# A linear-attention and two-network kernel: the last state update of the first planned body is moved to the border of two bodies

## What is computed

```python
k_n = k / (norm(k) + 1e-06)
for t in range(S):                      # S = 768
    y[:, :, t] = q[:, :, t] @ state
    v_old = k_n[:, :, t] @ state
    state = state + beta[t] * outer(k_n[:, :, t], v[:, :, t] - v_old)
h = x @ w_in                            # x: 3072 tokens x 384, w_in: 384 x 2048
g = where(h >= 1, h, where(h <= -1, 0, (h + 1) ** 2 / 4))
x2 = g @ w_out                          # 2048 x 384
xn = x2 / sqrt(mean(x2 * x2) + 1e-6) * rms_g
out = (silu(xn @ w_gate) * (xn @ w_val)) @ w_out2   # 384 x 1536 twice, 1536 x 384
```

## Time and profile before

| | us |
|---|---|
| median of 3 runs | 1040.0 |
| lowest and highest | 1039.98, 1040.58 |
| the profiled execution | 1040.48 |
| its span on the core | 1038.7 |
| PE busy in it | 1023.1 |
| DVE busy | 571.2 |
| ACT busy | 446.0 |

### The profile page before, as it was taken

The page is one execution under the profiler, slowest core; times in us unless marked ns, Lnnn a source line. Parts: engine busy times, 40 slices in busy tenths (PEclk is TensorE's granted clock), DMA queues, the critical chain, the costliest instruction groups (busy, mean ns, idle before and its releaser), DMA issues.

```text
span 1038.7 us, 25028 instructions
## 1 busy us (share of the span) xinstructions
PE 1023.1 (98%) x11080; PEld 845.6 (81%) x11080; DVE 571.2 (55%) x1098; ACT 446.0 (43%) x784; POOL 9.9 (1%) x19
## 2 busy tenths in 40 slices
PE   9999989999999999999999999999999999999998
PEld 4598888777777777777888888888888888888886
DVE  6878859778678777943466444234234333333322
ACT  7754645645544544553576442232232232232121
POOL 1000000000000000000000000000000000000000
PEclk9999999999999999999999999999999999999999
DMA  9204024013212402301512220200100100100101
GB/s 327 94 18 169 3 64 160 16 33 108 99 22 76 140 3 52 104 3 33 183 31 63 90 92 1 61 1 20 42 1 31 31 1 1 31 1 1 31 0 31
DMA packets 31211, 58.85 MB, mean 57 GB/s; under 512 B 2752, under 2 KB 21056, under 8 KB 29696
## 3 DMA queue, kind: packets, MB, share of 16 engines
q1 hardware_dynamic: 30656, 56.47, 17.5%
q10 hardware_dynamic: 448, 0.79, 0.3%
HBM read 43.88 MB, written 13.37 MB: 55 GB/s over the span
## 4 chain that ended last, share of the span: by engine, by line
PE 94%; ACT 2%; DVE 2%; issue 1%; DMA 1%; ACTq 0%
PE bank L805 22%; PE hps L1469 20%; PE acc L1487 19%; PE acc L833 11%; PE hps L805 7%; PE hps L833 4%; PE acc L1515 2%; PE bank L1347 1%; PE bank L1376 1%; PE bank L1395 1%; PE bank L1403 1%; PE bank L1421 1%; PE bank L1438 1%; PE bank L1335 1%; PE bank L1365 1%
## 5 line engine op out<-in xcount | busy, mean ns | idle before, releaser
L713 ACT ACTIVATE g<-bank 128x512 f32<-128x512 f32 x72 | 43.1, 599 | 242.1 <-PE bank L805 129.0
L1469 PE MATMUL hps<-xh,w1h 128*128 128x512 f32 (+1 forms) x336 | 127.7, 380 | 2.2 <-DVE g L1279 2.1
L1487 PE MATMUL acc<-g1h,w2h 128*128 128x512 f32 (+1 forms) x336 | 127.1, 378 | 0.4 <-issue 0.4
L1469 PE MATMUL hps<-xl,w1h 128*128 128x512 f32 (+1 forms) x336 | 122.0, 363 | 0.0
L1487 PE MATMUL acc<-g1l,w2h 128*128 128x512 f32 (+1 forms) x336 | 121.9, 363 | 0.0
L1487 PE MATMUL acc<-g1h,w2l 128*128 128x512 f32 (+1 forms) x336 | 121.8, 363 | 0.0
L1469 PE MATMUL hps<-xh,w1l 128*128 128x512 f32 (+1 forms) x336 | 121.8, 362 | 0.0
L1083 ACT ACTIVATE g1h<-g 128x512 fp32r<-128x512 f32 (+1 forms) x112 | 63.9, 571 | 128.2 <-DVE g L1279 113.0
L1074 ACT ACTIVATE g<-hps,half_c 128x512 f32<-128x512 f32 (+1 forms) x112 | 69.5, 621 | 68.7 <-PE hps L1469 67.3
L1287 DVE TENSOR_TENSOR g1l<-g,g1h 128x512 fp32r<-128x512 f32 (+1 forms) x112 | 68.4, 611 | 48.9 <-ACT g1h L1083 48.6
L1279 DVE SCALAR_TENSOR_TENSOR g<-hps,g 128x512 f32<-128x512 f32 (+1 forms) x112 | 68.2, 609 | 40.8 <-ACT g L1077 40.3
(11 more groups left out here) (238 smaller groups left out, 2026.7 us busy)
## 6 DMA issues: line engine op xcount, KB each, us to landing
kqT<-kq SPq DMA_DIRECT2D x11, 1024.0 KB, 7.1
v_in<-v SPq DMA_DIRECT2D x6, 768.0 KB, 5.3
k_in<-k SPq DMA_DIRECT2D x6, 768.0 KB, 5.3
x2d<-x2s SPq DMA_DIRECT2D x18, 256.0 KB, 5.5
x2t<-x2d SPq DMA_DIRECT2D x6, 768.0 KB, 5.4
y<-y_t SPq DMA_DIRECT2D x44, 96.0 KB, 2.2
x2d<-prob SPq DMA_DIRECT2D x20, 192.0 KB, 2.9
v_in<-x2d SPq DMA_DIRECT2D x10, 384.0 KB, 3.3
```

Source lines behind the costliest of these rows:

```text
L713: act.activation(silu[:, f % 2, :], gps[f % 2][:, :], ACT.Silu).then_inc(e_silu, 1)
L1469: last = pe.matmul(hps[f % 2][:, 0:WIDTH[n]], wt[:, kk, P * f:P * f + P], xx[:, kk, COLS[n]], start=(kk == 0 and e == 0), stop=(kk == KD - ...
L1487: last = pe.matmul(acc[j][:, 0:WIDTH[n]], wt[:, f, P * j:P * j + P], gg[:, f % 2, 0:WIDTH[n]], start=(f == 0 and e == 0), stop=(f == NF1 - ...
```

## The change

In body 1 the last unit of the chain, `KU 1 1`, is taken out of the even steps and given the due time 0.995, which is later than the last of the 192 groups. The remaining 17 units run from `lead` to 0.91 instead of 18 from `lead` to 0.89. In body 2 the two `GQ` units get the due times 0 and 0.09 instead of 0.04 and 0.09. `Z 1 1` and what follows it in body 1 stand 2.93 groups apart instead of 2.55. No instruction is added or removed. In body 2 the units from `Z 2 0` on stand 2.62 groups apart instead of 2.71; bodies 3 to 5 have the list they had.

```diff
--- before.py
+++ after.py
@@ -169,12 +169,15 @@
         at += w / (DENSE if k > 1 else 1.3 * LEAD if at * total < 36 else LEAD if turned is None else 2.5 * LEAD)
         if e == ("xd", k, 1):
             turned = at
-    lead, last = (turned, LAST - 0.02) if k == 1 else (at, LAST)
+    lead, last = (turned, LAST) if k == 1 else (at, LAST)
     us = solve(k) + serial(k)
+    if k == 1:
+        us.remove(("KU", k, HALVES - 1))
+        ev.append((0.995, ("KU", k, HALVES - 1)))
     if k == 1:
         ev += [((done + 68 + 10 * hf) / total, ("GQ", k, hf)) for hf in range(HALVES)]
     else:
-        ev += [(0.04 + 0.05 * hf, ("GQ", k, hf)) for hf in range(HALVES)]
+        ev += [((0.09 * hf if k == 2 else 0.04 + 0.05 * hf), ("GQ", k, hf)) for hf in range(HALVES)]
     begin = None
     for n, u in enumerate(us):
         ev.append((lead + (last - lead) * n / len(us), u))
```

## The result

| us | before | after |
|---|---|---|
| median | 1040.0 (5 runs, 1039.68 to 1041.07) | **1046.58** (5 runs, 1044.49 to 1047.23) |
| the profiled execution | 1040.48 | 1044.49 |
| its span | 1038.7 | 1042.7 |

The ratio is 1.0057, with a 95% interval of 1.0046 to 1.0068: slower, as forecast, but by 6.6 us where 2.8 were forecast, and outside the range of 1040.8 to 1045.0. The profiled execution is the fastest of the five. One execution lost 4.0 us against the profile of before, the median of five lost 6.6; both have to be explained.

A forecast was written before the change was run, and what follows sets the result against it. The prediction took PE as the bound, busy 1023.1 of 1038.7 us. Its terms, 4.1 - 2.1 + 0.35 + 0.7 = +3.05, rounded down to +2.8 on the median 1040.0, gave 1042.8 us, range 1040.8 to 1045.0.

The forecast's parts named there:

- The gap: Between `KU 1 1` and `GQ 2 0`: PE idles until the state addition, 4.1 us, bounds 2.45 and 4.9.
- The load: Output of `PU 1 1` coming back into `v_in`: store to load takes 3.3 us, arriving 8.0 after `PU 1 1`, holding `XE`.
- The clock: Rival, behind the idle time before `GQ 2 0`: the clock falls to half, losing 1.8 us more, 1044.6 us; chance 0.20.
- what it took back: Body 1: the new order costs +0.35 us by a longer wait before `U 1 1` and +0.7 by shifted code borders.
- The wider steps: Body 1: three groups of cover remove waits of 0.34, 0.38, 0.71, a 0.29 border and 0.4 of small things, -2.1 us.
- pairs side by side and to modelled ends: Small things in the gain: one unit edge of 0.19 less, idle times some 0.07 short each; 0.4 us, bounds 0 and 0.6.
- U 1 1: Before `U 1 1`: DVE has `sys` first, so the wait is 0.8 instead of 0.37; +0.35 us, bounds 0 and 0.8.
- the border after `KS 1 1` opens: Code border after `KS 1 1`, hidden so far, begins to cost; part of the upper bound of +1.5 us on code.
- The code borders: `GK 2 0`, `KS 1 0`, `QS 1 0`, `QS 1 1`: borders lie 6, 9, 12, 15 matmuls earlier; +0.7 us, bounds -1.5 and +1.5.
- The spread wins: Rival, dense part of body 1: extra room lets code arrive in time, -2.1 instead of +0.7 us, 1040.2 us; chance 0.15.
- The gap is short: Rival, before `GQ 2 0`: the load does not hold `XE`, idle 2.45 instead of 4.1 us, 1041.1 us; chance 0.15.
- the move would not bind: Rival, at the border: `GQ 2 0` need not wait for `KU 1 1`, 1038.7 us; given no chance.

The follow-up runs named there:

- e4: The changed kernel with only DVE's order altered: the state additions of `KU 1 1` come ahead of `XE`; median 1041.04 us, ratio 1.0003.
- e5: The changed kernel as it is, run and profiled a second time; median 1046.51 us, ratio 1.0058.
- e2: The kernel before with its old spacing, only `KU 1 1` moved last in body 1 and `GQ 2 0` first in body 2; median 1044.53 us, ratio 1.0033.
- e8: The kernel before with 16 more small warm-up matmuls at PE's start, which shifts the code borders; one run, 1042.88 us.
- e10: The kernel of e7 once more, unaltered; median 1039.9 us, ratio 0.9998.
- e1: The changed kernel with the wider steps alone: `KU 1 1` stays in the chain, `GQ 2 0` four groups into body 2; median 1041.91 us, ratio 1.001.
- e3: The changed kernel with 16 unused matmuls of 512 columns on PE between `KU 1 1` and `GQ 2 0`; median 1045.18 us, ratio 1.0043.
- e6: The changed kernel with `GQ 2 0` back at its old place, four groups into body 2; median 1043.07 us, ratio 1.0025.
- e7: The kernel before with one more group ahead of `GK 2 1`, `U 1 0` and `U 1 1`, border untouched; median 1040.49 us, ratio 0.9998.
- e9: e2 with only DVE's order altered: the state additions of `KU 1 1` come ahead of `XE`; median 1041.49 us, ratio 1.001.

## Why the prediction was wrong in size and right in direction

**The gap.** Right in mechanism, small in size: 4.6 and 4.8 where 4.1 was reckoned (bounds 2.45 and 4.9). Both sides of it fit: `KU 1 1` ends 8.25 after the end of `PU 1 1` (8.2 forecast), and from `XE` to `GQ 2 0` it is 161.28 - 157.10 = 4.18 (3.22 + 0.33 + 0.55 + 0.14 = 4.24 forecast). The load is what was sized wrong: from the issue of the store to that of the load it took 4.20, where the same half took 3.49 before. The step that took the value of the one half seen, with "no other transfer that I know of beside it", had no ground for the lower value: a packet of code came during the store in both kernels (last section). The prediction also expected the profile to name the state addition as what PE waits for; it names "issue", and e4 is what shows the addition.

**The clock: the step that failed.** The prediction gave the fall of the clock a chance of 0.20 and left it out of the time. It fell in each of the three profiles with a gap of over 2.3 us (after, e5, e2), and the mean clocks point to it in all nine runs of the change and in eight of nine of e2. The price of 1.8 for it was near in size (1.5 in the two profiles with 3.4 us of it). That the rival's 1044.6 is the profiled execution's 1044.49 is in part luck, as this execution lost the least to code of the six with this body 1. And the price was taken from one stay at half speed; the second profile has twice that and loses 2.7, and the mean clocks put at least two of the five timed runs there. Leaving the clock out of the sum is the largest part of the miss: in the second profile, whose time is near the median, it is 2.7 of the 3.8 us by which the forecast was short, the gap 0.7 (4.8 for 4.1), and the rest, the spread and what it took back, about 0.4. The argument against the rival, that small matmuls run right up to the gap, was worth nothing: they ran up to it in all three.

**The wider steps.** Of the 2.1, the waits of 0.38 and 0.71 went, as did the break of 0.29 in `KU 1 1`. The 0.34 before `GK 2 1` stayed, 0.32, although three groups stand there now. The rows show why: before, the code break of 0.43 stood behind the last matmul of `GK 2 0`, and ACT used it for its Gram copy; now it stands inside the unit and covers nothing. e8, with the break inside and still two groups, waits 0.68 there; e10, with a break of 0.72 behind the unit, not at all. From the start of A to the end of `PU 1 1` it is 35.12 before and 36.22 after, with six more groups in it, 6 x 0.356 = 2.14: the spread gained 1.0 there. The terms of the prediction for that stretch are -0.34 - 0.38 - 0.71 - 0.4 + 0.35 + 0.7 = -0.8. But this agreement is one execution's luck. The other five profiles with the same body 1 (e1, e3, e4, e5, e6) have 36.56 to 37.17, a gain of 0.1 to 0.7, and the mean of all six is **0.5**; by e1's median, which also has the late load in it, there is none.

**U 1 1.** Forecast 0.8 of waiting, measured 0.36, as before. The additional 0.35 did not come, because `KS 1 1` lost time to a code border of its own, 0.27 of idle time in a row that takes 1.59 from start to start instead of 1.08. DVE was free at 140.22, 2.84 after `KU 1 0` (forecast 2.9), and its subtraction then waited 0.16 more for the late `KS 1 1`. Without the break the wait before `U 1 1` would have been 0.36 + 0.51 - 0.16 = 0.7, an estimate from these rows. So one term's miss was another's hit: that break is the bound which the prediction named (the border after `KS 1 1` opens).

**The code borders.** The places came out as forecast: `GK 2 0` breaks with 6 matmuls left, `QS 1 0` with 45 instead of 33, `QS 1 1` with 27 instead of 12. PE's timeline of after has them, and the new one in `KS 1 1`:

```profile
121.79 0.34 PE L1338 MATMUL bank<-kqT 48*64 48x64 f32 x6 [0.43 <-issue]
...
132.15 0.88 PE L1406 MATMUL bank<-kqT,state 48*48 48x64 f32 x45 [0.31 <-issue]
...
139.97 0.37 PE L1379 MATMUL bank<-state,kqT 48*64 48x48 f32 x10 [0.27 <-issue]
...
145.47 0.65 PE L1406 MATMUL bank<-kqT,state 48*48 48x64 f32 x27 [0.76 <-issue]
```

The idle time in them, 0.43 + 0.31 + 0.27 + 0.76 = 1.77, is near that of before (0.43 + 0.80 + 0.87 = 2.10). e1, with the same places, has 0.35 + 0.84 + 0.51 + 1.04 = 2.74, so the low sum is one execution's luck in part.

**The rivals.** The clock was the case that came true. "The spread wins" fell with e1, which had neither gap nor clock and was not faster. "The gap is short" is what e2 has, by an earlier `PU 1 1`; even it was slower by 0.33% with the clock. That the move would not bind is excluded by e4 and e6, which changed the binding order and got 5.0 and 3.7 us of A back.

**The sum again.** In the first profile: gap 4.6, clock 1.5, spread -1.0, the break in `KU 1 1` -0.3, together 4.8, against 4.4 measured for A. In the second: 4.8 + 2.7 - 0.3 - 0.3 = 6.9, against 6.55. The 0.4 left both times is the size of what the prediction put down to pairs side by side and to modelled ends, but was not tested. Why half speed lasts 3.4 us in one run and 6.8 in another stays open. One slip in the prediction's chances changes nothing: the clock's 0.20 and nine tenths of 0.50 are 0.65 and not 0.66.

## What to carry to other kernels

Two units that depend on each other through another engine's queue should not stand side by side on PE: count everything that the other engine does first, here `XE`, `inv` and `g`, and put the short additions ahead of them (e4: 5.0 us back from a reordering of two operations on DVE). An idle time on PE like those here, 2.35 to 4.8 us, is to be priced with the clock behind it, 1.5 to 2.7 us more, and not alone. A stretch that differs by 1 us from one execution to the next is not to be read from one profile. Where a stretch is short of code or waits in a row for several things, a removed wait of 0.3 us is worth nothing until the measurement says otherwise.

## What the runs showed of the hardware

The granted clock fell after a gap of 2.35 us (e2), once PE had been back at work for 1.6 us, and once after a wait of 0.6 us only in a stretch of small matmuls (e7), in one of two profiles of that kernel. With idle times of at most 1.43 us on PE (e1, e4, e6, e9) none of the four profiles has it, and with the gap filled (e3) none of the four runs. Even the kernel before has it somewhere in about a quarter of its runs, by their mean clock, and those are 1.5 us longer.

From the issue of the two stores of `prob` to the issue of the load behind them, the same transfers took from 3.4 to 5.3 us. For `PU 2 1`, the changed kernel's and e3's timelines of the DMA queue:

```profile
239.66 0.82 SPq L876 DMA_DIRECT2D x2d<-prob  x2
243.11 0.38 SPq L881 DMA_DIRECT2D v_in<-x2d  x1
```

```profile
238.65 0.82 SPq L876 DMA_DIRECT2D x2d<-prob  x2
243.78 0.38 SPq L881 DMA_DIRECT2D v_in<-x2d  x1
```

The same store in the same place took 3.45 and 5.13. What differs is the code queue: in e3 a packet of 16 KB begins 2.8 us after the issue of the store and ends at 4.0, while the store is still under way; in after it begins at 3.0, and the store's last piece is done at 3.1. The twelve profiles hold 120 such round trips. In 78 a packet of code begins 0.3 to 3.3 us after the issue of the store, and they take 3.43 to 5.27, 34 of them 4.0 or more; the other 42 have none over 3.98, median 3.47. So code that comes in during the store goes with the long ones, though not every time, and this was seen and not tested. A chain with such a round trip in it and less than 2 us to spare is on the critical path in some kernels and not in others, and in e3 and e6 it took back 1.2 us of the gain of the experiment.

The Trainium skill (Runtime: NRT & Kernel Launch, Instruction fetch mechanics) has the crossing of a code block mostly hidden. The traces here show it hidden in body 2, where PE is busy for 60.00 of 60 us, and not among small matmuls, with breaks of 0.27 us (after) to 1.43 (e9).
